# Top-32 attention feeding a mixture of experts: the 24th score found in two search rounds, and the threshold's place marked on VectorE for the last two pairs

## What is computed

```python
scores = scale * np.matmul(q, k.transpose(0, 1, 3, 2))
kth = np.partition(scores, -top_k, axis=-1)[..., -top_k:-top_k + 1]   # top_k = 32
mask = scores >= kth
scores = np.where(mask, scores, -1000000000.0)
scores = scores - np.max(scores, axis=-1, keepdims=True)
attn = np.exp(scores)
attn = attn / (np.sum(attn, axis=-1, keepdims=True) + 1e-09)
return np.matmul(attn, v).astype(np.float32)
```

## Time and profile before

| | |
|---|---|
| median of 3 runs | 451.37 us (451.0 to 453.92) |
| the profiled execution | 452.31 us |
| its span, from the first to the last instruction | 450.5 us, so 1.81 us lie outside |
| mean granted TensorE clock | 0.986 of full speed |

### The profile page before, as it was taken

The page is one execution under the profiler, slowest core; times in us unless marked ns, Lnnn a source line. Parts: engine busy times, 40 slices in busy tenths (PEclk is TensorE's granted clock), DMA queues, the critical chain, the costliest instruction groups (busy, mean ns, idle before and its releaser), DMA issues. The chain is left out here.

```text
span 450.5 us, 8693 instructions
## 1 busy us (share of the span) xinstructions
PE 396.5 (88%) x2769; PEld 341.6 (76%) x2769; DVE 286.2 (64%) x1399; ACT 238.4 (53%) x428; POOL 232.8 (52%) x225
## 2 busy tenths in 40 slices
PE   2986779989799799897788999999999999999993
PEld 1553547867587687686677888878899999999792
DVE  2599999999999999999899966501020202122210
ACT  2233468987887888888798883123112122131320
POOL 4045468889889789899899814302011101020310
PEclk9999977999999999999999999999999999999998
DMA  4213142033060240232100108968999776777400
GB/s 104 55 41 66 26 123 55 1 68 108 8 167 2 46 129 0 67 127 94 28 1 2 28 3 276 360 224 259 393 320 327 244 261 207 254 255 242 174 22 21
DMA packets 56354, 58.44 MB, mean 130 GB/s; under 512 B 37102, under 2 KB 37102, under 8 KB 56304
## 3 DMA queue, kind: packets, MB, share of 16 engines
q1 hardware_dynamic: 54128, 53.10, 38.1%
q0 software_dynamic: 2176, 4.73, 2.9%
HBM read 45.99 MB, written 13.92 MB: 133 GB/s over the span
## 5 line engine op out<-in xcount | busy, mean ns | idle before, releaser
L515 POOL TENSOR_TENSOR rest<-below,scores 128x576 f32<-128x576 f32 x69 | 96.2, 1411 | 45.0 <-DVE below L1239 45.0
L705 PE MATMUL ps_o<-v_aug,pT 128*128 128x128 f32 (+2 forms) x800 | 100.9, 275 | 0.7 <-ACT pT L1050 0.7
L705 PEld LDWEIGHTS ps_o<-v_aug,pT 128*128 128x128 f32 (+1 forms) x800 | 93.9, 181 | 2.2 <-issue 1.3
L520 POOL TENSOR_TENSOR probs<-scores,probs 128x576 f32<-128x576 f32 x66 | 93.0, 1426 | 1.0 <-ACT probs L1026 1.0
L1140 ACT ACTIVATE scores<-ps_s 128x288 f32<-128x288 f32 x64 | 26.1, 411 | 104.8 <-PE ps_s L943 102.0
L1174 DVE MAX8 cand<-scores 128x8 f32<-128x96 f32 x432 | 72.4, 241 | 12.1 <-ACT scores L1000 12.0
L676 PE MATMUL ps_t<-ident,probs 128*128 128x128 f32 x360 | 54.7, 284 | 21.1 <-ACT pT L1050 15.2
L676 PEld LDWEIGHTS ps_t<-ident,probs 128*128 128x128 f32 x360 | 39.4, 143 | 36.2 <-issue 19.9
L943 PE MATMUL ps_s<-scores 128*128 128x192 f32 (+3 forms) x448 | 66.5, 306 | 0.0
L943 PEld LDWEIGHTS ps_s<-scores 128*128 128x128 f32 x448 | 64.4, 191 | 1.0 <-issue 0.7
L584 POOL DMA_INDIRECT out_dram<-yo,numbers x15 | 13.8, 919 | 96.7 <-DVE yo L1515 77.8
(11 more groups left out here) (156 smaller groups left out, 399.4 us busy)
## 6 DMA issues: line engine op xcount, KB each, us to landing
w_sb<-in_moe_w_dram SPq DMA_DIRECT2D x9, 2048.0 KB
scores<-in_moe_w_dram SPq DMA_DIRECT2D x7, 2048.0 KB, 13.0
dispatched<-empty SPq DMA_DIRECT2D x18, 257.0 KB, 4.0
scores<-dispatched SPq DMA_DIRECT2D x21, 192.8 KB
out_dram<-empty SPq DMA_DIRECT2D x9, 256.0 KB, 2.6
q_nat<-in_q_dram SPq DMA_DIRECT2D x16, 128.0 KB, 2.4
k_nat<-in_k_dram SPq DMA_DIRECT2D x16, 128.0 KB, 2.4
v_aug<-in_v_dram SPq DMA_DIRECT2D x16, 128.0 KB, 2.4
```

The costliest lines, as they stand in the source:

```text
L515: nc.gpsimd.tensor_tensor(rest[:, n % 3, :], below[:, n % 3, :], score_tile(n), ALU.mult).then_inc(rest_ready, 1)
L520: nc.gpsimd.tensor_tensor(probs[:, n % PROBS, 0:S], score_tile(n), probs[:, n % PROBS, 0:S], ALU.subtract).then_inc(masked_ready, 1)
L705: last = nc.tensor.matmul(dst, lhs, v_aug[:, g % 2, c, h, 0:width], start=(c == 0), stop=(c == TT - 1))
```

## The change

- The 24th score is found in two rounds. The two largest of each segment (the twelve "firsts") are no longer in the search of the upper scores. The eight largest of the firsts are taken as being above the 24th score; the four smallest firsts join the other 36 candidates, and of these 40 (in 42 columns, two of which are filled with a very low number) the sixteenth is the 24th of all: one MAX8, one MATCH_REPLACE8, one MAX8.
- The four smallest firsts come from `lowest_firsts`: a sign change of the 12 firsts of three tiles in one instruction, and a MAX8 over 12 elements for each tile. `join_lowest` turns their sign back. A `reduce_max` gives the highest score of each tile, which was `tops[..., 0]` before.
- The order within a group is new: `candidates`, `normalise`, `lowest_firsts`, `search_rest` of tile 0, `join_lowest`, `search_rest` of tile 1, `bounds`, `search_rest` of tile 2, `mark_below`.
- `count_bad` and `recheck` move from `candidates` into `bounds`, to after the first MAX8s and after the MATCH_REPLACE8s.
- In groups 18 to 23 VectorE computes `here` (three TENSOR_SCALAR over 8 elements), and GpSimd's `pick` is one instruction there in place of three.

```diff
-FIRST = TOP_K - 8
+SURE = 8
+LOW = 2 * SEGS - SURE
...
+            def pick_late(i):
+
+                g, tiles = tiles_of(i)
+                pool.wait_ge(here_late_ready, 3 * (i - PAIRWISE + 1))
+                pool.wait_ge(next_done, TILES * g + tiles.stop)
+                pool.wait_ge(thr_summed, i)
+                nc.gpsimd.tensor_tensor(picked8[:, tiles, :], here[:, tiles, :], next8[:, g % 2, tiles, :],
+                                        ALU.mult).then_inc(picked_ready, 1)
...
-                nc.scalar.activation(nmax[:, g % 2, tiles], tops[:, g % 2, tiles, 0], ACT.Copy, scale=-1.0).then_inc(edges_ready, 1)
+                nc.scalar.activation(nmax[:, g % 2, tiles], highest[:, g % 2, tiles], ACT.Copy, scale=-1.0).then_inc(edges_ready, 1)
...
+            def lowest_firsts(m, found):
 
                 g = m // 3
+                t = 3 * m % TILES
+                after(found)
                 if g >= 2:
                     dve.wait_ge(edges_ready, 2 * (g - 1))
...
+                turned = add(nc.vector.tensor_scalar(firsts[:, :, :, :], cand[:, :, 0:SEGS, 0:2], -1.0, None, ALU.mult))
+                add(nc.vector.reduce_max(highest[:, g % 2, t:t + 3], cand[:, :, 0:SEGS, 0], AX.X))
+                after(turned)
+                for j in range(3):
+                    last = add(nc.vector.max(lows[:, j, :], firsts[:, j, :, :].rearrange("p c k -> p (c k)")))
+                return last
+
+            def join_lowest(found):
+
+                after(found)
+                return add(nc.vector.tensor_scalar(cand[:, :, SEGS, 2:2 + LOW], lows[:, :, 0:LOW], -1.0, None, ALU.mult))
+
+            def bounds(m, joined):
+
+                g = m // 3
+                t = 3 * m % TILES
+                after(joined)
+                done = [add(nc.vector.max(upper[:, j, :], cand[:, j, :, 2:8])) for j in range(3)]
+                checked = [i for i in range(CHECKS) if m == (3 * i + 4 if i < PAIRWISE else i - PAIRWISE + ENDING + 2)]
+                counted = [count_bad(i) for i in checked]
+                for j in range(3):
+                    after(done[j])
+                    done[j] = add(nc.vector.match_replace(left[:, j, :, :], upper[:, j, :], cand[:, j, :, 2:8], NEG))
+                for i, seen in zip(checked, counted):
+                    recheck(i, seen)
+                for j in range(3):
+                    after(done[j])
+                    done[j] = add(nc.vector.max(tops[:, g % 2, t + j, :], left[:, j, :, :]))
                 for j in range(3):
                     bounded[j] = done[j]
...
+            def mark_places(m):
+
+                for j in range(3):
+                    n = 3 * m + j
+                    t = n % TILES
+                    dve.wait_ge(below_ready, n + 1)
+                    nc.vector.tensor_scalar(here[:, t, :], places[:, :], count[:, n // TILES % 2, t:t + 1], None,
+                                            ALU.is_equal).then_inc(here_late_ready, 1)
...
                 if m < GROUPS:
-                    bounds(m, found)
+                    lows_found = lowest_firsts(m, found)
...
                 if m > 0:
-                    search_rest(m - 1)
+                    search_rest(m - 1, 0)
+                if m < GROUPS:
+                    joined = join_lowest(lows_found)
+                if m > 0:
+                    search_rest(m - 1, 1)
+                if m < GROUPS:
+                    bounds(m, joined)
+                if m > 0:
+                    search_rest(m - 1, 2)
...
+                if ENDING <= m < GROUPS:
+                    mark_places(m)
```

More of the change, by code:

```diff
@@ L95, in routed_topk_attention_moe @@
         scores = sb("scores", [P, HELD * S])
-        cand = sb("cand", [P, 3, SEGS * 8])
-        left = sb("left", [P, 3, SEGS * 8])
-        tops = sb("tops", [P, 2, TILES, FIRST])
+        cand = sb("cand", [P, 3, SEGS + 1, 8])
+        firsts = sb("firsts", [P, 3, SEGS, 2])
+        lows = sb("lows", [P, 3, 8])
+        upper = sb("upper", [P, 3, 8])
+        left = sb("left", [P, 3, SEGS + 1, 6])
+        tops = sb("tops", [P, 2, TILES, 8])
+        highest = sb("highest", [P, 2, TILES])
         below = sb("below", [P, 3, S])
@@ L226, in routed_topk_attention_moe @@
         here_ready = sem("here_ready")
+        here_late_ready = sem("here_late_ready")
         picked_ready = sem("picked_ready")
@@ L1173, in candidates @@
                         part = score_tile(n)[:, c * (S // SEGS):(c + 1) * (S // SEGS)]
[L1174 to L1181, removed]
@@ L1182, in candidates @@
-                return found
-            def bounds(m, done):
+                        last = add(nc.vector.max(cand[:, j, c, :], part))
+                return last
+            def lowest_firsts(m, found):
                 g = m // 3
+                t = 3 * m % TILES
+                after(found)
                 if g >= 2:
                     dve.wait_ge(edges_ready, 2 * (g - 1))
[L1189 to L1200, removed]
+                turned = add(nc.vector.tensor_scalar(firsts[:, :, :, :], cand[:, :, 0:SEGS, 0:2], -1.0, None, ALU.mult))
[3 more added lines that the diff above has]
+                    last = add(nc.vector.max(lows[:, j, :], firsts[:, j, :, :].rearrange("p c k -> p (c k)")))
+                return last
@@ L1210, in push_down_last, with search_rest @@
                     nc.vector.tensor_tensor(rest[:, j, :], below[:, j, :], score_tile(n), ALU.mult).then_inc(rest_ready, 1)
[L1212 to L1220, removed]
+            def search_rest(m, j):
+                n = 3 * m + j
+                t = n % TILES
+                dve.wait_ge(rest_ready, n + 1)
+                if m >= 6 and t % 3 == 0:
+                    dve.wait_ge(picked_ready, check_of(n - 2 * TILES) + 1)
+                nc.vector.max(next8[:, n // TILES % 2, n % TILES, :], rest[:, j, :]).then_inc(next_done, 1)
             def sum_picked(i):
@@ L1238, in mark_below @@
                         dve.wait_ge(rest_ready, n - 2)
-                    nc.vector.tensor_scalar(below[:, j, :], score_tile(n), tops[:, g % 2, t, FIRST - 1:FIRST], 0.0,
+                    nc.vector.tensor_scalar(below[:, j, :], score_tile(n), tops[:, g % 2, t, 7:8], 0.0,
                                             ALU.is_lt, ALU.add, accum_out=count[:, g % 2, t:t + 1]).then_inc(below_ready, 1)
+            def mark_places(m):
+                for j in range(3):
+                    n = 3 * m + j
+                    t = n % TILES
+                    dve.wait_ge(below_ready, n + 1)
+                    nc.vector.tensor_scalar(here[:, t, :], places[:, :], count[:, n // TILES % 2, t:t + 1], None,
+                                            ALU.is_equal).then_inc(here_late_ready, 1)
             def find_bad(i):
@@ L1433, in _ @@
             nc.vector.memset(r_hot[:, :, TT, :], 0.0)
+            add(nc.vector.memset(cand[:, :, SEGS, :], NEG))
             nc.vector.memset(ps_o[:, :, :], 1.0).then_inc(psum_clean, 1)
```

7 lines of the change are left out of this document (4 added, 3 removed).

## The result

The kernel became slower: 468.4 us (median of 4 runs, 467.76 to 468.8) against 451.72 (4 runs of the kernel before on the same chip), a ratio of 1.036 with a 95% interval of 1.033 to 1.039. The forecast was 442.8. The profiled execution has a span of 466.0 us where that of before had 450.5, so 15.5 us more. In experiment 10 four of the twelve runs were slower than the rest of the same kernel, one of them with 671 us, and its ratio leaves them out.

A forecast was written before the change was run, and what follows sets the result against it. VectorE was taken to bound attention up to about 245 us, with TensorE behind it. Gains of 6.95 and 1.9 us made 8.85, rounded to 8.6: 442.8 us from 451.37, range 440.3 to 447.0.

The forecast's parts named there:

- the pricing of the join (0.08 us) and of the marks: VectorE's small sign change and three marks per group priced by length, each bounded by 0.06 and 0.23 us.
- Rival (b): VectorE's small instructions wait for GpSimd, 0.73 us each: a loss of 20 to 33 us, 471 to 484; chance 0.07.
- The search's own arithmetic: VectorE's two-round search costs 1.67 us a group against 2.06, saving 0.39; a group of about 9.3 us.
- The check's read: VectorE's read of the check's DMA, placed about 3 us later in the group, loses all four waits.
- ScalarE's stand at `edges`: ScalarE waits some 2 us once per pair for the later recheck; costed at zero as it has idle time.
- rival (a): The delay at edges does not fit and ScalarE sets the pair's time: gain 4.5 to 6.5, 445 to 447 us; chance 0.15.
- the 8.85 us: Whole forecast gain: 6.95 us up to GpSimd's start of group 20 plus 1.9 in the ending, rounded down to 8.6.
- 6.95: GpSimd starts group 20 earlier by this many us: 3.5 + 3.1 from the search, 0.8 from the check, less 0.45 for marks.
- Moving the check: On VectorE, count_bad and recheck later in the group remove the DMA waits, 0.81 us counted; the move costed at zero.
- The ending: GpSimd's groups 20 and 21 with the one-instruction pick take 21.0 us in place of 22.92, gaining 1.9 us.
- a wait that I named only as a way to be wrong: VectorE waiting for a score tile, listed among the signs that would show the forecast wrong; no size given.

The follow-up runs named there:

- experiment 10: The changed kernel with the marks undone and the join reading 15 dense elements, writing five by three strided: 449.1 us, 0.991 of the kernel before.
- experiment 5: The changed kernel with marks nine wide, read three by three from rows of four and written densely, join unchanged: 456.67 us, 1.010.
- experiment 3: The changed kernel with the marks comparing against a constant in place of each row's count: 463.66 us, 1.027.
- Experiment 4: The changed kernel without the marks, its first sign change writing with the same strides as it reads: 462.69 us, 1.025.
- experiment 1: The changed kernel with the marks alone undone (GpSimd's pick is three instructions again), the two-round search kept: 453.66 us, 1.004.
- experiment 9: The changed kernel with marks nine wide from rows of four, and the join reading 15 dense elements, writing five by three strided: 448.52 us, 0.991.
- experiment 8: The changed kernel with marks nine wide from rows of four and the join in the form that also writes a sum: 446.3 us, 0.989.
- experiment 11: The kernel of experiment 9 with the check's read and recheck back in candidates, after the second and third tile: 447.8 us, 0.991.
- experiment 7: The changed kernel with both the join and the marks in the form that also writes a sum: 445.97 us, 0.987.
- experiment 2: The kernel before, with its three-round search, plus the marks alone: 466.03 us, 1.032.

## Why the prediction was wrong

**The step that failed** is the pricing of the join (0.08 us) and of the marks (0.075 each, 0.23 a group). I put both on the line of MAX8 and of L1424 and bounded each by 0.06 and 0.23 us. Neither was a row of a plain TENSOR_SCALAR beside GpSimd's elementwise instructions, so the bounds could not hold the case that mattered. Measured: the join a mean of 0.490 and up to 1.01 us (3.50 in experiment 5), the marks a mean of 1.220. The range should have gone up to GpSimd's own instruction, 1.39 us for each small one, since 2.78 for two stands in the earlier trace rows.

**Rival (b) was the truth, and its weight of 0.07 was the error of judgement.** I took L1424's 0.281 us for 128 elements, which lies on MAX8's line of 0.98 ns an element, as evidence against the collision. The marks and joins wait all the same, whatever their rate: with 8 or 12 elements (0.158 us for a mark of experiment 3 that did not wait, 0.152 for such a join) a doubled rate would hardly show. L1424 says nothing about it, because four of its eight instructions run with GpSimd idle and the other four beside its scatter DMAs, none beside its elementwise instructions. I noted that "no row here shows that form beside GpSimd" and yet priced it as if one did. The page that I set aside said what happens: the Trainium skill ("SBUF — State Buffer", two separate sides) has the two engines exclude one another for a whole instruction. For VectorE waiting for GpSimd the trace agrees, to 0.05 us for the join that ends at 126.44; the other direction can't be seen with instructions this short. Of the two pages only the doubled rate is not seen, in the row of L1424.

**Rival (b)'s size was off in both directions.** It priced 0.73 us a piece, from 1.55 against 0.817, and hit all three places: 29 us for the sign changes and 13 for the marks, 471 to 484. In truth the first sign change is spared altogether; the join waits long in ten groups only (0.72 to 1.01 us; 0.15 to 0.17 where GpSimd is idle or just between two instructions, as in groups 0 to 6); the marks wait 1.0 each in the mean and not 0.73, since nearly each has to wait for a gap of its own. 18.0 + 8.1 is 26.1 in place of 42, and the kernel came out at 468.4.

**Which small instruction is spared** was not asked at all. Experiment 4 shows that it is by the pair of patterns: 18 pairs of two, read with a stride and written densely, are spared; the same, read and written with the same stride, are not. The Trainium skill has this too ("VectorE: DVE Perf Modes", What auto-detection actually checks: an instruction is taken for the doubled mode if the outermost dimensions that are not one are both even or equal), and the six patterns tried agree with it: 8 onto 8, 3 x 4 onto 3 x 4 and 3 x 6 x 2 onto itself wait, while 3 x 6 x 2 onto a dense 36, 3 x 3 onto a dense 9 and a dense 15 onto 5 x 3 do not. A simpler rule, by which any difference between the two patterns spares the instruction, would agree with the six as well; no pair that differs and is even on both sides was tried. What the rows add is the price at these sizes: in groups 0 to 4, with GpSimd idle, the first sign change lasts 0.185 us with equal patterns (experiment 4) and 0.191 with unequal ones (experiment 1), so there are some 6 ns to win and up to 1.3 us to lose.

**What was right.** The search's own arithmetic: where the join is spared a steady group takes 9.29 to 9.34 us (119.65 to 128.97 in experiment 9 is 9.32), as forecast, against the 9.72 of the earlier trace rows. The check's read has no wait left (idle 0.0 in its line), as forecast. From the pick of group 21 to that of group 22, with no idle time, GpSimd takes 9.81 us in experiment 9 (225.35 to 235.16), for which I had 9.82. ScalarE's stand at `edges` is there, 1.77 us for the "some 2 us" that I expected:

```profile
147.65 0.21 ACT L1033 ACTIVATE edge<-thr 128x9 f32<-128x9 f32 x1 [1.77 <-DVEq L1325]
```

In experiment 9 these waits are 1.05, 1.71 and 0.43 us in three of the pairs and none in the others, and VectorE waits for no score tile behind group 4. So rival (a), in which ScalarE sets the pace, did not come.

**How much of the 8.85 us arrived.** The medians of the cured kernels, 446 to 449, are 3.1 to 5.5 us below the kernel before on their chips. The profiled execution of experiment 8 ends its span at 441.4 us, 9.1 less than before, but that it meets the forecast is in part luck. It is the fastest of its four runs (443.22 us, against their median of 446.3), and it is set against an execution that lies 0.94 us above its median. By stages it is 5.2 us early at the pick of group 20 (212.20), where I had 6.95; 6.7 at that of group 22 (233.58), where I had 8.85; and 7.55 at the `rden` (273.89). The last 1.55 us come behind it, where the change touches nothing.

**Two smaller steps were wrong in size.** Moving the check was to take away waits of 0.81 and 1.55 us, of which 0.81 stands in the sum, and was costed at zero; the waits are gone, but 2.7 us of new idle time have come, which experiment 11 removes. The ending was to bring 1.9 us, from 22.92 to 21.0; in experiment 9 it is 1.5, to 21.44. What is missing is in group 20, 11.63 us in place of 11.18: the short pick is over before `mark_below` has its first result, and GpSimd stands 0.44 us for it (experiment 9, at 214.38), a wait that the three small instructions had covered.

**And a wait that I named only as a way to be wrong** is there: VectorE waits for a score tile in group 4. VectorE at that place in experiment 7, in the kernel before, and in experiment 2:

```profile
55.65 2.02 DVE L1191 MAX8 cand<-scores 128x8 f32<-128x96 f32 x12 [2.88 <-ACT scores L1019]
```

```profile
52.09 2.15 DVE L1174 MAX8 cand<-scores 128x8 f32<-128x96 f32 x12
```

```profile
55.23 1.06 DVE L1187 MAX8 cand<-scores 128x8 f32<-128x96 f32 x6 [2.11 <-ACT scores L1013]
```

But the change is not its cause. Experiment 2 has the old search and does nothing new before group 18; its VectorE begins group 4 at 52.06, as before, and it waits all the same. The tiles are made by TensorE at this point. In the kernel before eight matmuls take 1.19 us there, in experiment 2 the same eight take 2.15 and come 1.1 us later:

```profile
51.26 1.19 PE L656 MATMUL ps_s<-kT,qT 64*64 64x288 f32 x8
```

```profile
52.35 2.15 PE L669 MATMUL ps_s<-kT,qT 64*64 64x288 f32 x8
```

All twelve traces of other kernels have this wait, eleven with 1.55 to 2.92 us and experiment 8 with 0.79; the one trace of the kernel before has none. So a comparison with that one execution makes the others look up to 3 us worse than the change made them. Whether other executions of the kernel before have the wait no trace tells, so how much of the missing gain it explains stays open, and so does why TensorE works at about half its rate there in some executions and not in others.

## What to carry to other kernels

Before a small plain elementwise instruction on fp32 data in SBUF is priced by its length, look at what GpSimd does beside it: here one of eight elements cost up to the whole of GpSimd's instruction (1.4 us), and one of twelve once nearly three of them (3.5 us), on the engine that set the pace. Such an instruction is spared if input and output have patterns that do not match (here an odd outermost dimension on one side, dense on the other) or if it is written in the summing form; both turned a loss of 3.6% into a gain of about 1%. A rival for which only "no row shows this form under this condition" can be said against it deserves more than a small chance: a row of the same instruction without the neighbour is no evidence. And a wait that a profile shows after a change and not before belongs to the change only if it is absent where the changed part can't act yet.

## What was not expected of the hardware

- Very small instructions wait as well: 8 elements, 0.219 us when free, 1.220 in the mean beside GpSimd.
- A pointer operand is not why the instruction waits, but with it each one of a row waited anew: three in 3.93 us, with a constant in 2.58.
- An instruction that waits can miss gaps between GpSimd's back-to-back instructions: 3.50 us across three masks.
- The marks wait most, because they stand right behind the instruction that sets GpSimd going. GpSimd then stands idle itself (5.12 us) until VectorE comes, so the two engines take turns where they had overlapped.
- The summing form of the same instruction, on the same buffers and patterns, does not wait: 148 ns against 490, 216 against 1220.
